# Seven quarter products for layer two's first product, in two token passes

## The reference

```python
x = attention(q, k, v)                  # 1536 tokens x 512
h = x @ w_in                            # layer one, 512 -> 1024
solu = h * softmax(h)
x2 = (normalize(solu) * g_ln) @ w_out   # 1024 -> 512
h = x2 @ w2_in                          # layer two, 512 -> 2048
r = np.maximum(h, 0.0)
out = (r * r) @ w2_out                  # 2048 -> 512
```

## Time and profile before

| | us |
|---|---|
| three runs, median (lowest to highest) | 483.92 (483.8 to 483.97) |
| the profiled execution's span, first to last instruction | 481.6 |
| around the span, from the median | 2.3 |
| PE busy | 471.1, 98% |
| DVE busy | 278.1, 58% |
| ACT busy | 212.9, 44% |
| POOL busy | 103.8, 22% |

### The profile page before, as it was taken

One profiled execution on the slowest core, in us unless ns is written; L12 is line 12 of the kernel. 1 busy time (PEld: TensorE's weight loads), 2 busy tenths in 40 slices (PEclk: granted clock), 3 DMA queues, 4 the chain that ended last, 5 costly groups with the idle time before them and its releaser, 6 DMA issues.

```text
span 481.6 us, 7337 instructions
## 1 busy us (share of the span) xinstructions
PE 471.1 (98%) x2634; PEld 382.5 (79%) x2634; DVE 278.1 (58%) x514; ACT 212.9 (44%) x559; POOL 103.8 (22%) x155
## 2 busy tenths in 40 slices
PE   7889999999999999999999999999999999999997
PEld 5667787887788888878888888888888888888885
DVE  3899889898989888767755354322222233222232
ACT  3677777656777666242324253222222232222221
POOL 2366323231321232739930000000000000000000
PEclk9999999999999999999999999999999999999999
DMA  7931437765569424498400000200000020000002
GB/s 214 315 92 50 136 85 215 205 192 159 149 180 219 113 57 120 119 252 240 90 1 0 1 0 1 87 0 0 0 0 0 0 87 1 0 0 1 0 1 87
DMA packets 51990, 41.80 MB, mean 87 GB/s; under 512 B 28088, under 2 KB 38072, under 8 KB 51448
## 3 DMA queue, kind: packets, MB, share of 16 engines
q1 hardware_dynamic: 51192, 40.74, 29.9%
q10 hardware_dynamic: 768, 0.66, 0.5%
HBM read 30.38 MB, written 11.01 MB: 86 GB/s over the span
## 4 chain that ended last, share of the span: by engine, by line
PE 91%; DVE 3%; POOL 2%; ACT 1%; DMA 1%; issue 1%; ACTq 0%; DVEq 0%; POOLq 0%
PE score_ps L1675 27%; PE h_ps L1689 14%; PE w_ps L1516 13%; PE h_ps L1476 12%; PE w_ps L1689 7%; PE wt_ps L1689 7%; PE o_ps L1438 4%; PE score_ps L1404 2%; PE wt_ps L1404 2%; PE wt_ps L1415 1%; DMA x2T<-qT 1%; PE o_ps L1459 1%; POOL pT_own L576 1%; PE w_ps L1541 1%; DVE prob L1095 1%
## 5 line engine op out<-in xcount | busy, mean ns | idle before, releaser
L1675 PE MATMUL score_ps<-x2T_hi,w2in_hi 128*128 (+1 forms) x192 | 74.8, 389 | 0.0
L1675 PE MATMUL score_ps<-x2T_hi,w2in_lo 128*128 (+1 forms) x192 | 74.7, 389 | 0.0
L1675 PE MATMUL score_ps<-x2T_lo,w2in_hi 128*128 (+1 forms) x192 | 74.7, 389 | 0.0
L1328 DVE TENSOR_TENSOR e<-e 128x512 f32<-128x512 f32 x24 | 17.9, 744 | 82.0 <-ACT e L968 82.0
L1328 DVE TENSOR_TENSOR sq<-relu 128x512 f32<-128x512 f32 x24 | 17.2, 717 | 77.0 <-ACT relu L968 77.0
L968 ACT ACTIVATE relu<-score_ps 128x512 f32<-128x512 f32 x24 | 14.3, 597 | 90.5 <-PE score_ps L1675 90.5
L968 ACT ACTIVATE e<-score_ps 128x512 f32<-128x512 f32 x24 | 14.4, 599 | 89.7 <-PE score_ps L1675 89.7
L1675 PEld LDWEIGHTS score_ps<-x2T_lo,w2in_hi 128*128 128x128 f32 x192 | 36.0, 188 | 7.5
L1675 PEld LDWEIGHTS score_ps<-x2T_hi,w2in_hi 128*128 128x128 f32 x192 | 36.1, 188 | 7.5
L1675 PEld LDWEIGHTS score_ps<-x2T_hi,w2in_lo 128*128 128x128 f32 x192 | 36.0, 188 | 7.4
L742 ACT ACTIVATE prob<-sm,nbias 128x132 f32<-128x132 f32 (+1 forms) x96 | 37.6, 393 | 4.1 <-DVE nbias L1019 3.4
(11 more groups left out here) (192 smaller groups left out, 1095.0 us busy)
## 6 DMA issues: line engine op xcount, KB each, us to landing
u_dram<-uT SPq DMA_DIRECT2D x18, 256.0 KB, 3.2
lnT_raw<-u_dram SPq DMA_DIRECT2D x36, 128.0 KB, 2.9
w2in<-w_in SPq DMA_DIRECT2D x4, 1024.0 KB, 5.3
w2out<-w_out SPq DMA_DIRECT2D x8, 512.0 KB, 9.9
V<-v SPq DMA_DIRECT2D x12, 256.0 KB, 3.2
x2T<-x_dram SPq DMA_DIRECT2D x12, 256.0 KB, 4.8
x_dram<-x SPq DMA_DIRECT2D x44, 64.0 KB, 2.2
k_raw<-kT SPq DMA_DIRECT2D x20, 132.0 KB, 2.9
```

The costliest lines, as they stand in the source:

```text
L1328: nc.vector.tensor_tensor(sq[f % 2], relu[f % 2], relu[f % 2], ALU.mult).then_inc(sq_ready, 1)
L1675: done = mm(h2_ps[f % 2], ws[:, c, fs], xs[:, c, bass.ts(blk, BLK)], start=(c == 0 and i == 0), stop=(c == MC - 1 and i == 2))
```

## The change

Layer two's first product is done by one level of Strassen's method (in Winograd's form). The input (512 channels x tokens of a pass) and the weights (512 x 256 hidden units: chunk j and chunk j + 8) are cut into quarters, and seven products of quarter size replace eight. The tokens go in two passes of 768 (`TS`), in halves of 384 (`TH`), and each pass has 8 iterations (`NJ`), 16 in all (`NI`). An iteration has seven products `multiply(i, n)` of 6 matmuls (2 chunks, 3 terms) with 384 columns, and 12 output units of `project2(i - 1)`, 3 matmuls of 512 columns each, spread between them. Two PSUM banks hold the products. Products that belong together are added in a bank; the others are combined by DVE: ACT copies the first product to p1 and takes the ReLU of the upper left quarter (`corner`), DVE makes u2 and u3 (`sum_2`, `sum_3`), `lower_right`, `lower_left` and `upper_right`, gates (`gate_corner`, `gate_sum`) and splits (`split_g`). ACT makes the high parts, as before.

The combinations of the input (T1 to T4) are made by POOL for the first pass (three of them in step t = 9 of layer one, behind `inverse_std(9)`) and by DVE for the second, in iterations 2 to 6, one to three instructions of 128x768 each. POOL makes the four sums of each weight tile and all its low parts. The weights of layer two are fetched a tile at a time, once for each pass. The outputs have six PSUM banks. At the handover `project(9)` has 8 of its 24 matmuls ahead of the hidden products and 16 behind; `project(10)` writes to o_ps; and the loops of layer two are written out.

```diff
+PASSES = 2
+TS = T // PASSES
+TH = TS // 2
+NJ = C2 // 2
+NI = PASSES * NJ
+A11, A12, A22, S1, S2, S3, S4 = range(7)
+B11, B21, B22, T1, T2, T3, T4 = range(7)
+PRODUCTS = ((A11, B11, 0, True), (S2, T2, 1, True), (A12, B21, 0, False), (S3, T3, 1, False),
+            (S1, T1, 0, True), (A22, T4, 1, False), (S4, B22, 0, False))
...
@@ POOL, in the loop over t @@
+                if t == NT - 3:
+                    sum_x(T1, 0, x_quarter(0, 1), x_quarter(0, 0))
+                    sum_x(T2, 1, x_quarter(1, 1), x_combination(0, T1))
+                    sum_x(T3, 1, x_quarter(1, 1), x_quarter(0, 1))
...
+            pool.wait_ge(scored, PAIRS * NT)
+            sum_w2(0)
+            split_w2_first(0)
+            split_w2_sums(0)
+            split_w2_last(0)
+            split_x(B21)
+            split_x(T3)
+            inverse_std(NT - 1)
+            pool.wait_ge(xc_split[T2], 1)
+            sum_x(T4, 3, x_quarter(1, 0), x_combination(0, T2))
+            for i in range(1, NI):
+                sum_w2(i)
+                split_w2_first(i)
+                split_w2_sums(i)
+                split_w2_last(i)
...
@@ ACT @@
+            for i in range(1, NI):
+                copy_p1(i)
+                round_g(i - 1, 2)
...
+                round_wy(i)
+                if i + 1 < NI:
+                    round_w2(i + 1)
+                corner(i)
+                round_g(i, 0)
+                if i + 1 < NI:
+                    round_w2_sums(i + 1)
...
+                round_g(i, 1)
...
@@ DVE @@
+            def upper_right(i):
+                dve.wait_ge(multiplied, NP * i + 7)
+                nc.vector.tensor_tensor(gated[:, 3, :], prod_ps[0], u2[:, :], ALU.add).then_inc(added, 1)
...
+                lower_left(i)
+                gate_sum(i, 1)
+                if i == 2:
+                    sum_x(T1, 0, x_quarter(0, 1), x_quarter(0, 0))
+                    sum_x(T2, 1, x_quarter(1, 1), x_combination(1, T1))
+                elif i == 3:
+                    sum_x(T3, 2, x_quarter(1, 1), x_quarter(0, 1))
+                    split_x(1, B11)
+                elif i == 4:
+                    split_x(1, T2)
+                    split_x(1, B21)
+                elif i == 5:
+                    split_x(1, T3)
+                    split_x(1, T1)
+                    dve.wait_ge(xc_split[T2], 2)
+                    sum_x(T4, 3, x_quarter(1, 0), x_combination(1, T2))
+                elif i == 6:
+                    split_x(1, T4)
+                    split_x(1, B22)
...
+                upper_right(i)
+                split_g(i, 1)
+                gate_sum(i, 2)
...
@@ PE @@
-                project(n - 2, 0, 24)
+                project(n - 2, 0, 8)
                 pe.wait_ge(u_ready, 2 * n)
                 hidden(n, 0, 24)
+                project(n - 2, 8, 24)
...
+            def multiply(i, n):
...
+                if n == 0 and i:
+                    pe.wait_ge(added, 5 * i)
...
+                for c in range(2):
+                    for k in range(3):
+                        ws, xs = ((w2_hi, xc_hi), (w2_hi, xc_lo), (w2_lo, xc_hi))[k]
+                        done = mm(prod_ps[bank], ws[i % 2][:, wk, c, :], xs[s][xk][:, c, :], start=(opens and c == 0 and k == 0),
+                                  stop=(c == 1 and k == 2), skip_group_check=True)
...
+            multiply(0, 0)
+            multiply(0, 1)
             project(NT - 2, 0, 24)
+            multiply(0, 2)
+            multiply(0, 3)
             transpose_ln(NT - 1)
+            multiply(0, 4)
+            project(NT - 1, 0, 12)
+            multiply(0, 5)
             project(NT - 1, 12, 24)
+            multiply(0, 6)
+            for i in range(1, NI):
+                multiply(i, 0)
+                multiply(i, 1)
+                project2(i - 1, 0, 2)
+                multiply(i, 2)
+                multiply(i, 3)
+                project2(i - 1, 2, 5)
+                multiply(i, 4)
+                multiply(i, 5)
+                project2(i - 1, 5, 8)
+                multiply(i, 6)
+                project2(i - 1, 8, 12)
+            project2(NI - 1, 0, 12)
```

More of the change, by code:

```diff
@@ L529, in side_loads @@
+            for i in range(2, NI):
+                load_wy(i)
+                if i + 1 < NI:
+                    load_w2(i + 1)
+                if i == NJ + 2:
+                    store_y(0)
+            store_y(1)
+            sp.wait_ge(y_stored, 16 * (PASSES * YT + 1))
         def side_loads(act):
@@ new lines, in corner, with round_g @@
+            def corner(i):
+                act.wait_ge(multiplied, NP * i + 3)
+                if since(i, 1):
+                    act.wait_ge(g_split, 3 * i - 2)
+                nc.scalar.activation(gated[:, 0, :], prod_ps[0], ACT.Relu).then_inc(corner_ready, 1)
+            def round_g(i, part):
+                tiles = (slice(0, 1), slice(1, 3), slice(3, 4))[part]
+                act.wait_ge(gated_ready, 3 * i + part + 1)
+                nc.scalar.activation(g_hi[i % 2][:, tiles, :], gated[:, tiles, :], ACT.Copy).then_inc(g_rounded, 1)
@@ L956, in _, with copy_y @@
+            def copy_y(s, qs):
+                for q in qs:
+                    act.wait_ge(y_done, YT * s + q + 1)
+                    nc.scalar.copy(y[:, q, :], y_ps[q]).then_inc(y_copied_act, 1)
             for part in range(len(LN_PARTS)):
@@ L1368, in _ @@
+            split_g(NI - 1, 2)
+            copy_y(1, (1, 3, 5))
         @block.tensor
@@ new lines, in project2 @@
+            def project2(i, first, last):
+                j, s = i % NJ, i // NJ
+                for n in range(first, last):
+                    tile, r, q = UNITS[n]
+                    if n == 0:
+                        pe.wait_ge(wy_split, i + 1)
+                    if n % QH3 == 0:
+                        pe.wait_ge(g_split, 3 * i + (1, 2, 2, 3)[tile])
+                    if i == 0 and n == 2 * QH3:
+                        pe.wait_ge(x2_squared, NT)
+                    if s and j == 0 and r == q // QH3:
+                        pe.wait_ge((y_copied_act, y_copied_dve)[q % 2], q // 2 + 1)
+                    rows = slice(q % QH3 * P, (q % QH3 + 1) * P)
+                    for k in range(3):
+                        gs, ws = ((g_hi, wy_hi), (g_hi, wy_lo), (g_lo, wy_hi))[k]
+                        done = mm(y_ps[q], gs[i % 2][:, tile, rows], ws[i % 2][:, r, :],
+                                  start=(j == 0 and r == q // QH3 and k == 0), stop=(j == NJ - 1 and r != q // QH3 and k == 2))
+                    if j == NJ - 1 and r != q // QH3:
+                        done.then_inc(y_done, 1)
+                    elif n == len(UNITS) - 1:
+                        done.then_inc(projected, 1)
```

531 lines of the change are left out of this document (313 added, 218 removed).

## The result

The changed kernel takes **489.22 us** (median of 4 runs, 488.61 to 490.01), the kernel before 483.86 beside it: ratio 1.0118, 95% interval 1.0102 to 1.0134. It is 1.2% slower, and the forecast of 490.0 holds. Its terms hold less well: 7.4 us of costs that no term had stand against 7.5 us that the forecast waits were too long, so that the number is partly luck.

The account below looks back on a forecast made before the run. TensorE, busy 98% of the span, was taken as the bound. Terms -14.0 + 5.4 + 6.1 + 8.6 = +6.1 took the span from 481.6 to 487.7 us; with 2.3 outside it, 490.0, range 475 to 495.

Parts of the forecast that it names:

- Point 1: Layer two's first product: 576 matmuls of 512 columns at 0.2267 us become 672 of 384 at 0.1735; -14.0 us.
- Point 4: Step t = 9 of layer one: POOL's three sums delay DVE's u halves and xT_lo, so TensorE waits; +5.4 us.
- half clock: TensorE's clock falls in step t = 9's gap: 2 us more, 492; outside the sum, inside the range and first case.
- Point 5: Handover to layer two: project(10) 2.0 us late, last tile's lnT 3.6, next m0 0.8; +6.1, bounds 0 and 9.
- Point 6: Iterations 2 to 6: next first product waits for upper_right behind x instructions, four times 1.4 and once 3.0; +8.6 us.
- around the span: Time outside the profiled span: the three runs' median lies 2.3 us above it, carried over to the forecast.
- Point 2: One layer-two iteration: 15.45 us on TensorE; POOL 8 us, DVE 7.5, ACT some 6, so by shares nothing is full.
- Point 3: POOL and DVE lock each other out of SBUF, taking turns by whole instructions; DVE instructions with a PSUM operand aren't held.
- partly hidden case: Rival on the waits: turns fall luckier, say half of 20.1 us of waiting, giving 480; chance 0.25.
- Weight loads: Rival on TensorE's products: 672 loads of 188 ns set the pace, +9.7 us on any case, alone 480; chance 0.04.
- pass two's x: Rival for iteration 2: the load of pass two's input comes 5 us too late, giving 495; chance 0.04.

Follow-up runs that it names:

- run 4: Changed kernel with weight transfers (from tile 10), POOL's work (tile 12) and DVE's and ACT's work on hidden units (iteration 14) cut in steps: 488.41 us.
- run 8: Changed kernel, but from iteration 9 on TensorE makes all seven products first, then the twelve output units in one piece: 495.67 us.
- run 9: Changed kernel with three reordering edits together, plus output weights of iterations 10 to 15 moved to SBUF addresses at multiples of 4096: 475.81 us.
- run 10: Changed kernel, but from iteration 10 on layer two's POOL, DVE and ACT instructions (except output copies) work on 2 columns, weight transfers cut to 64 KB: 487.56 us.
- run 11: Changed kernel with three reordering edits together, plus output weights of iterations 10 to 15 placed 1344 bytes past multiples of 2048: 476.05 us.
- run 1: Changed kernel, but POOL starts its three sums of step t = 9 only after DVE has finished xT_lo of tile 10: 483.97 us.
- run 5: Changed kernel with the two SBUF buffers of the hidden units' high parts swapped, and the two of their low parts too: 488.67 us.
- run 6: Changed kernel, handover reordered: DVE's splits of T4 and B22 later, upper_right of iteration 0 earlier, last 6 matmuls of project(11) behind the seventh product: 484.73 us.
- run 2: Changed kernel, but in iterations 2 to 6 DVE's instructions on pass two's input stand behind the last gate_sum instead of ahead of upper_right: 484.2 us.
- run 3: Changed kernel with POOL's weight work in iterations 2 to 6 cut to 2 of 128 columns of each piece, DVE's order unchanged: 484.38 us.

## Why the prediction was right, point by point

| term | forecast | measured | shown by |
|---|---|---|---|
| 1. products | -14.0 | -14.0 at 0.1735, and +3.1 that no term had | periods; runs 4, 8 to 11 |
| 4. step t = 9, wait | +5.4 | +4.35 | run 1 |
| 4. half clock | left out (rival, 2) | +2.7 | run 1 |
| 5. handover | +6.1 | +4.9, 1.6 of it half clock | runs 5, 6 |
| 6. iterations 2 to 6 | +8.6 | +4.9 | runs 2, 3 |
| sum, in the span | +6.1 | +6.0 of 6.7 | |
| around the span | 2.3 | 1.7 | profiled execution |

Measured 0.7 us more in the span than the terms hold; 0.37 of it is there before step t = 9, the rest I can't place. The profiled execution is the slowest of the four (490.01), and the kernel before has 2.2 to 2.3 around its span where the changed one has 1.7; so the medians are only 5.4 apart.

**What kept the number.** The waits of points 4, 5 and 6 came out 1.05, 2.8 and 3.7 us shorter than forecast, 7.5 in all. The half clock (2.7 and 1.6) and the longer pace (3.1) add 7.4 that the sum had at nothing. The direction and the places follow from the mechanism; that the total is right within 1 us is luck.

**Point 1** took one pace for all matmuls of a shape. The 384 columns came out as interpolated between the earlier trace rows, 0.1733 in a clean group. But I carried 0.2267 over to the second product, "which stays at 576 matmuls", and its matmuls stand 0.230 to 0.2333 apart: (15.66 - 15.45) x 15 = 3.1 us. The saving was thus 10.9. By the formula of the Trainium skill (TensorE: Matmul & The Clock Gate, Back-to-back issue gap) for an isolated matmul, 384 columns would have 162.5 ns, an estimate; the trace has 173.3 at best, 11 above, as with 512.

**Point 2** adds POOL's work up to 8 us an iteration; its own terms give 7.4. Nothing hangs on it.

**Point 3, the lock**, is right and is the cause of the waits. Run 3 shows it by itself for iterations 2 to 6: 0.95 against 1.49, and the waits gone with the order unchanged. Run 1 shows it for step t = 9, where only the time of POOL's sums was changed. At the handover it is read from the stretched rows; run 6 changes the order alone. That an operand in PSUM frees DVE holds for all 80 instructions of L1487 to L1504. The Trainium skill (SBUF — State Buffer, SBUF: two separate sides) states this lock; the trace agrees (0.95 against 1.49).

**Point 4** has the mechanism instruction by instruction. The wait was 1 us less: PE went on at 184.70, 0.37 late from before, where I had 185.4; the third sum ended at 183.7, and I had 184.25. What failed is leaving the clock out of the sum: the earlier trace rows had a price for it, 2 us, and it cost 2.7 behind an idle time of 3.6 us.

**Point 5** had project(10) 2.0 late and it was 0.4. POOL's low part of the sums ended 2.8 us ahead of layer two's first product, at 209.27 against 212.10; I had reckoned 1.85, and everything of DVE behind it moved by that. project(11) waited 2.3 (forecast 3.6) and m0(1) 0.9 (forecast 0.8). The half clock there, 1.6, was not foreseen.

**Point 6** has the right place, and the largest wait at i = 5, and is off in size: i = 2 cost 1.3 (forecast 1.4), but i = 3, 4 and 6 cost 0.5 each, and i = 5 cost 1.9 (forecast 3.0). Measured from m0(5) at 301.84, gate_sum ended at 12.7 instead of 13.1, the x instructions stood 1.42 apart instead of 1.6, and upper_right of two x instructions would end at 16.0 instead of 16.8: 0.5 of wait, not 1.4. My turn was the sum of both lengths, 0.7 + 0.9; in the trace the next one gets in some 0.1 to 0.2 before the recorded end of the other.

**The rivals.** The partly hidden case was right about the sizes of point 6, and the waits in all came to 12.6 us instead of 20.1; clock (4.3 in all) and pace (3.1) on the other side kept the total up. Weight loads did not set the pace, and pass two's x was not late.

## What to carry to other kernels

Before work is given to an idle GpSimd, look at what VectorE does beside it: where both worked from SBUF here they took turns, and a stretched instruction on VectorE's path to a matmul became a TensorE wait. Instructions of VectorE with an operand in PSUM were free of it. The remedy was order, not less work: the same 607 DVE and 241 POOL instructions cost 13 us less when the held ones had slack behind them. A wait of TensorE of 2 to 4 us can bring a half clock behind it, here 1.6 to 2.7 us more, and should be priced with that as a risk, not as a certainty.

## What was not expected of the hardware

- TensorE's pace depends on where its moving operand lies in SBUF: 36 matmuls of 512 columns took 8.38 us with rows 1536 bytes past a multiple of 2048, 8.39 at multiples of 4096, and 8.29 at 1344 past, as the hidden units' own buffers (runs 9 and 11). In the last twelve units, which no product interrupts, it was 0.2336 at multiples of 4096 and 0.2264 at 1344 past. Of the 8.29, 0.09 above run 8's 8.20 is what the first matmuls behind each product cost. Why the place matters, and which offsets besides these three are good, stays open.
- The half clock is not settled by the length of the wait. A wait of 3.6 to 3.7 us in step t = 9 had it behind it in all eight traces that have the wait, for 6.8 us in five and 3.4 in three. The wait of 2.1 to 2.3 us at the handover had it, for 3.4 us, in six of eight traces and not in the other two (runs 5 and 10). The wait of 1.8 us behind iteration 5 never had it, in seven traces. What decides between them no run here shows.
